# Chunked delta-rule attention: four 64x64 TensorE tiles by a crossed token side, 16x16 substitution with two merge levels, inverses two chunks ahead

## The reference

```python
B, H, S, D = q.shape            # 4, 8, 768, 48
k_n = k / (norm(k, axis=-1) + 1e-06)
state = zeros((B, H, D, D))
for t in range(S):
    y[:, :, t] = einsum('bhd,bhde->bhe', q[:, :, t], state)
    v_old = einsum('bhde,bhd->bhe', state, k_n[:, :, t])
    state = state + beta[t] * einsum('bhd,bhe->bhde', k_n[:, :, t], v[:, :, t] - v_old)
```

## Time and profile before

| what | us |
|---|---|
| median of three runs | 1134.25 |
| the profiled execution, its own time | 1137.29 |
| its span | 1135.5 |
| attention, from the start to the last logits copy | 449.3 |
| routing, experts and gated MLP, the rest of the span | 686.2 |
| PE busy in the whole span | 902.7 |
| DVE busy | 499.8 |
| ACT busy | 336.9 |
| POOL busy | 109.6 |

### The profile page before, as it was taken

The page is one execution under the profiler, slowest core; times in us unless marked ns, Lnnn a source line. Parts: engine busy times, 40 slices in busy tenths (PEclk is TensorE's granted clock), DMA queues, the critical chain, the costliest instruction groups (busy, mean ns, idle before and its releaser), DMA issues. The chain is left out here.

```text
span 1135.5 us, 24072 instructions
## 1 busy us (share of the span) xinstructions
PE 902.7 (79%) x10426; PEld 830.6 (73%) x10426; DVE 499.8 (44%) x834; ACT 336.9 (30%) x571; POOL 109.6 (10%) x121
## 2 busy tenths in 40 slices
PE   0229705895598997359999559999999999999997
PEld 0128704885598997259999548888888888888886
DVE  3772395357828312646666434532232322322322
ACT  1203201332123223035555253523223213232211
POOL 0401100102001000024334300000000000000000
PEclk9999655887678688669999869999999999999999
DMA  9303200331112112296666420020020100100101
GB/s 236 74 1 82 68 21 2 86 100 44 57 46 71 59 44 82 91 363 220 227 215 213 147 83 1 1 57 1 1 56 1 30 26 0 28 0 0 28 1 28
DMA packets 26709, 82.01 MB, mean 72 GB/s; under 512 B 4320, under 2 KB 16736, under 8 KB 23936
## 3 DMA queue, kind: packets, MB, share of 16 engines
q1 hardware_dynamic: 24192, 73.26, 21.0%
q0 software_dynamic: 2432, 7.47, 2.1%
HBM read 63.42 MB, written 17.30 MB: 71 GB/s over the span
## 5 line engine op out<-in xcount | busy, mean ns | idle before, releaser
L1246 PE MATMUL pg<-xT,wg 128*128 128x512 f32 x648 | 165.0, 398 | 1.7 <-DVE xT L1178 1.7
L1230 PE MATMUL po<-wo,hh 128*128 128x384 f32 x864 | 163.7, 337 | 0.1
L1246 PE MATMUL pv<-xT,wv 128*128 128x512 f32 x648 | 159.0, 390 | 0.0
L1230 PEld LDWEIGHTS po<-wo,hh 128*128 128x128 f32 x864 | 153.1, 188 | 5.6 <-DVE hh L1190 0.4
L1188 DVE TENSOR_TENSOR hf<-pv,sil 128x512 f32<-128x512 f32 x72 | 49.8, 692 | 227.2 <-PE pv L1246 200.8
L1246 PEld LDWEIGHTS pv<-xT,wv 128*128 128x128 f32 x648 | 122.0, 188 | 26.2
L1246 PEld LDWEIGHTS pg<-xT,wg 128*128 128x128 f32 x648 | 121.1, 190 | 26.4 <-DVE xT L1178 3.0
L1137 ACT CAST hh<-hf 128x512 fp32r<-128x512 f32 x72 | 44.7, 621 | 152.2 <-DVE hf L1188 152.2
L1133 ACT ACTIVATE sil<-pg 128x512 f32<-128x512 f32 x72 | 43.2, 600 | 150.8 <-PE pg L1246 150.8
L444 PE MATMUL pzx<-T,Q 32*32 32x32 f32 x768 | 16.9, 205 | 86.4 <-DVE T L362 53.2
L444 PEld LDWEIGHTS pzx<-T,Q 32*32 32x32 f32 x768 | 15.5, 120 | 88.9 <-DVE T L362 53.8
(11 more groups left out here) (178 smaller groups left out, 1155.5 us busy)
## 6 DMA issues: line engine op xcount, KB each, us to landing
w1s<-in_w SPq DMA_DIRECT2D x9, 1536.0 KB, 7.5
w2s<-in_w SPq DMA_DIRECT2D x9, 1536.0 KB
kT<-in_kT SPq DMA_DIRECT2D x24, 192.0 KB, 6.3
ktok<-in_ktok SPq DMA_DIRECT2D x12, 384.0 KB, 8.0
qT<-in_qT SPq DMA_DIRECT2D x24, 192.0 KB, 3.8
vt<-in_vtok SPq DMA_DIRECT2D x12, 384.0 KB, 5.6
x_gather<-xs SPq DMA_DIRECT2D x24, 192.0 KB, 1.9
x_next<-xs SPq DMA_DIRECT2D x24, 192.0 KB, 2.1
```

The lines of the kernel that those rows point to most:

```text
L1230: ins = nc.tensor.matmul(po[j][:, 0:DM], a[:, j * 128:(j + 1) * 128], w[:, f, :], start=(f == 0 and n == 0), stop=(f == K2 - 1 and n == 2))
L1246: ins = nc.tensor.matmul(ps[:], a[:, k, c], x[:, k, :], start=(k == 0 and n == 0), stop=(k == KD - 1 and n == 2))
```

## The change

1. **Crossing.** On the token side (k, v, beta by token, and y, R, U, Q, P, A) the heads with odd u have their two halves exchanged (`halves` on the host, `crossed` in the kernel). A matmul that reads channels and writes tokens then goes from side e to side e ^ u % 2, so four neighbouring matmuls lie on all four 64x64 tiles. Even and odd u write to different PSUM banks (pairs pY, pB, pS). The loop goes over whole chunks, and DVE and ACT operations over the columns of one parity.
2. **Inverse.** DVE substitutes 16x16 blocks: 14 steps instead of 30, on operands of 28 to 112 elements per partition. Two merges follow, 16 to 32 (`merge1`, `merge2`, added by DVE in `merge_out`) and 32 to 64 (`blocks_zx`, which does z of chunk n and x of chunk n - 1 together).
3. **Order.** Inverses run for two chunks at a time, two chunks ahead of their use; grams run six chunks ahead (`LEAD`). The first two grams, inverses and merges come before the rest of the prologue. beta has a semaphore of its own and is the first load; the routing weights wr are loaded later.
4. POOL clears P's and Q's blocks; the large memset of P on DVE is gone.

The diff, cut to its core:

```diff
-BATCH = (2, 4, 4, 2)
-SHARE = (0.5, 1.5, 4.5)
-NORM_AT = {2: 3, 5: 4, 9: 5}
+LEAD = 6
+SHARE = (3.0, 1.2, 1.3, 0.5)
+NORM_AT = {0: 3, 2: 4, 4: 5}
...
-            load_k(0)
-            sp.dma_start(beta[:], beta_d).then_inc(s_small, 16)
+            sp.dma_start(beta[:], beta_d).then_inc(s_beta, 16)
+            for c in range(4):
                 load_k(c)
             load_qv(0)
-            sp.dma_start(wr[:], wroute_d).then_inc(s_small, 16)
+            sp.wait_ge(s_red, 2)
+            sp.dma_start(wr[:], wroute_d).then_inc(s_wr, 16)
```

In DVE's substitution and the additions of the merges:

```diff
-                for j in range(1, BLK - 1):
-                    w = BLK - 1 - j
+                for i in range(1, 15):
+                    w = 15 - i
...
+            def merge_out(c):
+                dve.wait_ge(s_m2, c + 1)
...
+                v.tensor_tensor(block_, second, block_, ALU.add)
+                for t in range(2):
+                    block_ = T[c // 2 % 2][low(t), t0:t0 + NP, 0:w]
+                    ins = v.tensor_tensor(block_, first[low(t)], block_, ALU.add)
+                ins.then_inc(s_m2e, 1)
```

On DVE before the loop:

```diff
-            v.memset(P[:].rearrange("p s u i -> p (s u i)"), 0.0)
-            dve.wait_ge(s_small, 32)
+            dve.wait_ge(s_beta, 16)
             norm(0)
+            gram_out(0)
+            gram_out(1)
+            advance(invert(0), 1000.0)
             norm(1)
+            merge_out(0)
+            gram_out(2)
+            merge_out(1)
+            gram_out(3)
             norm(2)
+            gram_out(4)
+            gram_out(5)
+            work = invert(1)
```

On DVE in the loop, behind U:

```diff
+                advance(work, SHARE[1] if c else 1000.0)
+                if c == 0:
+                    work = invert(2)
+                if c + 2 < NC:
+                    merge_out(c + 2)
+                advance(work, SHARE[2])
+                if c + LEAD < NC:
+                    gram_out(c + LEAD)
+                advance(work, 1000.0 if c % 2 else SHARE[3])
```

On PE, and on the host (last two lines):

```diff
+            def crossed(out, lhsT, rhs, us=range(NP)):
+                for u in us:
+                    for e in range(2):
+                        ins = nc.tensor.matmul(out(u)[half(e ^ u % 2)], lhsT(u, e), rhs(u, e), start=True, stop=True)
+                return ins
...
+            def merge1(c):
...
+                for u in range(NP):
+                    for q in range(4):
+                        rows = slice(BLK * q, BLK * q + w)
+                        ins = nc.tensor.matmul(pzx[BLK * q:BLK * q + BLK, u * w:u * w + w], Q[rows, s, u, 0:BLK],
+                                               T[c // 2 % 2][rows, c % 2 * NP + u, 0:w], start=True, stop=True)
...
+                pe.wait_ge(s_q, 2 * min(c + LEAD, NC))
+                if c:
+                    pe.wait_ge(s_se, 2 * c)
+                    pe.wait_ge(s_y, 4 * c)
+                crossed(lambda u: pY[u % 2][:, col(u, D)], lambda u, e: kT[half(e, D), sk, u],
+                        lambda u, e: St[half(e, D), u]).then_inc(s_rf, 1)
...
+        y = x.reshape(2, 2, H, NC, C, -1).copy()
+        y[:, :, 1::2] = y[:, ::-1, 1::2].copy()
```

More of the change, by code:

```diff
@@ L127, in attention, with half, low, high @@
         block = ctx.enter_context(nc.Block())
[L129 to L152, removed]
+        def half(i, rows=HALF):
+            return slice(i * HALF, i * HALF + rows)
+        def low(t):
+            return slice(t * HALF, t * HALF + BLK)
+        def high(t):
+            return slice(t * HALF + BLK, t * HALF + 2 * BLK)
+        def units(p, x):
+            return x.rearrange("p (i two) n -> p i two n", two=2)[:, :, p]
+        def bank(x, n):
+            return x[:, 0:8 * n].rearrange("p (i n) -> p i n", n=n)
+        def gram_banks(c):
+            return pY if c < LEAD and c % 2 else pB
         @block.sync
@@ L302, in _ @@
+            for h in (2 * NC - 2, 2 * NC - 1):
+                turn(h)
+                logits_out(h)
         @block.vector
@@ L466, in _ @@
             pe.wait_ge(s_const, 4)
-            for c in chunks_of(0):
-                for g in range(2):
-                    gram(c, g)
-            pe.wait_ge(s_small, 32)
-            z_part(0)
-            for h in range(2 * NC):
-                c, g = divmod(h, 2)
+            gram(0)
+            gram(1)
+            gram(2)
+            gram(3)
+            pe.wait_ge(s_zp, 1)
+            merge1(0)
+            merge2(0)
+            blocks_zx(0)
+            merge1(1)
+            merge2(1)
@@ L474, in _, with col @@
+            blocks_zx(1)
+            gram(4)
+            gram(5)
+            pe.wait_ge(s_wr, 16)
+            for c in range(NC):
                 sk, sq_ = c % KRING, c % QRING
-                units = grams(h)
-                us = range(g * 8, g * 8 + 8)
+                def col(u, w):
+                    return slice(u // 2 * w, u // 2 * w + w)
+                pe.wait_ge(s_q, 2 * min(c + LEAD, NC))
                 if c:
-                    pe.wait_ge(s_se, h - 1)
-                pe.wait_ge(s_a, h)
@@ new lines, in _ @@
+                pe.wait_ge(s_r, 2 * c + 2)
+                for u in range(NP):
+                    for e in range(2):
+                        ins = nc.tensor.matmul(pY[u % 2][half(e), col(u, D)], qT[half(e, D), sq_, u],
+                                               St[half(e, D), u], start=(u < 2), stop=False, skip_group_check=True)
+                ins.then_inc(s_y1, 1)
+                if c and c + 2 < NC:
+                    merge1(c + 2)
+                if c:
+                    logit(2 * c - 2)
@@ L535, in _ @@
+                if c and c + 2 < NC:
+                    merge2(c + 2)
+                pe.wait_ge(s_u, 2 * c + 2)
+                for u in range(NP):
+                    for e in range(2):
+                        t = e ^ u % 2
+                        ins = nc.tensor.matmul(pS[u % 2][half(e, D), col(u, D)], ktok[half(t), sk, u], U[half(t), u],
+                                               start=(c == 0 and u < 2), stop=(c == NC - 1 and u >= NP - 2),
                                                skip_group_check=True)
@@ L536, in _ @@
                 ins.then_inc(s_df, 1)
[L537 to L547 removed]
+                pe.wait_ge(s_y1, c + 1)
@@ new lines, in _ @@
+                for u in range(NP):
+                    for e in range(2):
+                        t = e ^ u % 2
+                        ins = nc.tensor.matmul(pY[u % 2][half(e), col(u, D)], AT[half(t), u], U[half(t), u],
+                                               start=False, stop=(u >= NP - 2), skip_group_check=True)
+                ins.then_inc(s_yf, 1)
+                if c == 0:
+                    merge1(2)
+                if c + LEAD < NC:
+                    gram(c + LEAD)
+                if c == 0:
+                    merge2(2)
```

526 lines of the change are left out of this document (276 added, 250 removed).

## The result

The changed kernel takes 1121.29 us (median of 7 runs, 1115.59 to 1122.80) against 1131.75 for the kernel before (7 runs, 1126.73 to 1135.58): ratio 0.988, 95% interval 0.985 to 0.991. Forecast were 989 us and a range of 945 to 1090. The direction was right; of the 145 us expected 10 came. The last logits copy stands at 434.5 us instead of 449.1, and the stages behind it are unchanged.

A forecast was written before the change was run, and what follows sets the result against it. PE's work at a mostly split clock and DVE's substitutions were taken to bound the attention. 64+37+5x20+4x18+15+13+3 = 304 us against 449.3, 145 less, gave 989 us (chance 0.50), range 945 to 1090.

The forecast's parts named there:

- 20 us per chunk: Attention loop, chunks 1 to 5: 17.2 us of PE work at clock 0.75 plus 2.8 us of waits per chunk.
- clock of 0.75: PE's granted clock in the loop, kept from 300 to 449 us before: 13.4 us per chunk becomes 17.2.
- Bound: Attention, slices 1 to 16: PE's work at a mostly split clock and DVE's substitutions set its time; largest hole 44.9 us.
- Crossing, 15.8 ns per load: 64-column products on four tiles: half of 31.6 ns per load, 1.01 us per whole-chunk product where two halves took 2.03.
- Rival A: Loop products: crossed tiles don't overlap, chunks 1 to 5 take 27.5 us, total 1071 us, 1109 with slow merges; chance 0.28.
- Six such: PE's chunk: k St, k q', q St, P R, A U and gram all cross, 6.1 us together at the full clock.
- Merges 4.4 us: PE's merge1, blocks_zx and merge2 per chunk: 1.09, 1.09 and 2.18 us with four row quarters at once.
- Rival C: Loop: small merge matmuls and handover waits keep the clock at 1.2 GHz, 26 us per chunk, total 1057 us; chance 0.12.
- Substitution: DVE's inverses: 28 steps at 0.29 us, three transposes at 1.9 and memsets 0.3, 14.1 us per two chunks.
- Prologue: Before the loop: the 15.28 us wait and memset go, invert(0) ends at 35.7, the loop starts at 64, not 80.7.
- Chunk 0: Loop's first chunk: DVE's norm(3) and invert(1) after U delay merge1(2) to gram_out(6); it ends at 101, 37 us long.
- Sum: Attention: prologue and chunk times add to 304 us against 449.3, 145 less, giving 989 us for the kernel.

The follow-up runs named there:

- e6: Changed kernel plus 96 unread full-size bf16 matmuls per chunk (32 each behind merge1, merge2 and k q'): 1128.37 us, ratio 0.9972 to the kernel before.
- e9: Changed kernel without its merge levels, DVE substituting whole 32x32 blocks, swap and order kept: 1065.71 us, ratio 0.9402 to the kernel before.
- e1: Changed kernel with only the swap of the odd heads (the crossing) undone: 1135.68 us, ratio 1.0028 to the kernel before.
- e2: Changed kernel with merge1 and merge2 done for only 1 of 16 units: 1038.61 us, ratio 0.9169 to the kernel before.
- e8: Changed kernel with the earlier kernel's late start, DVE waiting for wr before its first norm: 1134.56 us, ratio 1.0012 to the kernel before.
- e5: Changed kernel with the swap undone and merge1 and merge2 done for only 1 of 16 units: 1065.15 us, ratio 0.9435 to the kernel before.
- e13: Changed kernel without merge levels (DVE substitutes 32x32 blocks) and with the swap undone: 1091.12 us, ratio 0.9611 to the kernel before.
- e3: Changed kernel with merge1 and merge2 moved together behind the chunk's products: 1132.49 us, ratio 0.9976 to the kernel before.
- e4: Changed kernel plus 24 unread full-size bf16 matmuls per chunk, 8 at each of three places: 1127.84 us, ratio 0.9947 to the kernel before.

## Why the prediction was wrong

The step that failed is the 20 us per chunk: its clock of 0.75, kept from the kernel before, first of all, then its six crossed products, and a term for PE's code that was not there. A chunk took 30.4 us.

- **Bound.** Right that DVE's substitution and PE's work set the pace. Not asked: what feeds PE. The trace of before had a packet per 6.9 us in the loop, and so nothing to see but 2.2 us of pauses.
- **Crossing, 15.8 ns per load: right.** 1.84 us for 64 loads at 1.2 GHz is 28.8 ns, and e6 has 1.05 us at the full clock, 16.4 ns. Rival A falls: two tiles of one row half do work at once. The rule of the Trainium skill ("TensorE: Matmul & The Clock Gate", Part 3) that stood beside it, overlap only where the row group differs, does not agree with this trace: straight and crossed products change between the row halves alike, and only the crossed ones take half the time (1.84 against 3.56 us).
- **"Six such": wrong.** Four products cross, besides the update. q St (L610) and P R (L623) read and write the same side and take 3.56. That is 2.0 us per chunk at the full clock, and could be read in the kernel's code.
- **Merges 4.4 us: right in work** (1.80, 3.60 and 1.93 at 1.2 GHz, 4.1 at the full clock by the factor 1.8), wrong in what they are: 448 of 910 recorded matmuls per chunk. The price of the level that the change adds is 5% of the kernel (e9), 56 us, not 2.2 us per chunk.
- **Clock 0.75: wrong, the largest term.** It was 0.53 and 0.50. Work of 15.4 instead of 13.4, times 1.8, is 27.7; the groups of a chunk sum to 27. With 2.6 us of pauses for code that makes the 30.4 us from one state copy to the next. Against my 20: 2.6 from the two products, 8.0 from the clock, the pauses in place of the handovers. The clock fell with both parts of the change (e1, e2); why, no run shows.
- **Rival C (1057)** described the trace best, PE busy all along at 1.2 GHz, but had not the two products, the pauses and the start; its chance was 0.12. The time also missed its sum by 64 us. What the high clock alone would have brought is open: e6 had it only with 79 us of added matmuls, and there the idle time rose by 23 us.
- **Substitution** 14.1: it took 16 (49.3 us in 5 pairs for the steps, 29.1 for the transposes, 1.8 for the memsets). Not on the path in the later chunks.
- **Prologue:** the inverse ended at 37.6 (35.7 forecast), the loop started at 72.8 (64): z(0) took 5.0 us instead of 1.7 with a 3.1 us pause for code in it, and the gram outputs ended at 72.7. **Chunk 0** took 47.0 us, not 37: invert(1) ended at 102.2, since U came 12 us late. The hole of 15.17 us there was forecast as up to 16.
- **Sum.** Start 9, chunk 0 10, the rest 112 us too little (119.8 to 434.5 instead of 101 to 304). The loop itself got 6.7 us shorter where some 129 were forecast, and e8 without the early start is level with the kernel before: the right direction owes much to a side part of the change.

## What to carry to other kernels

Beside busy time and clock, count instructions: packets of the instruction queue per stretch, times the shortest spacing seen, are a floor under every stretch of small matmuls (3.2 us per 128 recorded matmuls in the traces here). Before work is moved from one engine to many small matmuls, compare that floor with the forecast; pauses inside one line with "issue" behind them are its sign. And when a change has two parts, the one that adds instructions can eat what the other saves.

## What the runs showed of the hardware

- Four 64x64 tiles work at once when the columns alternate within a row half: 28 ns per load at 1.2 GHz against 55 with two tiles, and 16.4 ns at the full clock (e6).
- PE's code arrives in 16 KiB packets, never less than 3.2 us apart in any trace here, though a packet itself takes about 1.1 us (median; 1.92 us for the one at 210.93), and PE goes on 1.2 to 1.6 us behind its landing. Why the packets do not follow each other more closely is open.
- The granted clock fell with the swap (0.63 to 0.52), though PE was about as busy (188 and 180 of 200 us), and as much without the merges (e5 0.74, e2 0.63). It fell with the merges too (e2 0.63 to 0.52). In the kernels with one merge level the swap made little difference (e13 0.65, e9 0.63 in the loop). It rose to 0.83 with 96 full-size bf16 matmuls per chunk. What sets it I leave open: e3 and e4 hardly moved it, and no run separated it from the pauses.
